# Pooled q and k rows of batch 1: summed by VectorE in place of TensorE's products with the identity

## The reference, cut to what matters

```
def sm_attn(qq, kk, vv):
    s = scale * qq @ kk^T ; s = s - max(s) ; a = exp(s) ; a = a / (sum(a) + 1e-9)
    return a @ vv
# q, k, v: [4 batches, 8 heads, 576 tokens, 64]; factor = 4
q_d = q.reshape(B, H, 144, 4, D).mean(axis=3)     # k_d and v_d likewise
out_up = np.repeat(sm_attn(q_d, k_d, v_d), 4, axis=2)
# local part: each token sees the tokens within +-3 of it
attn_out = out_up + out_local
x = attn_out, heads merged                          # [2304 tokens, 512]
x = (x @ w_a * (x @ w_b)) @ w_out                   # 512 -> 1536 -> 512
h = x @ w_in ; solu = h * softmax(h) ; out = layernorm(solu) * g_ln @ w_out2
```

## Time and profile before

| what | value |
|---|---|
| median of 3 runs | 773.45 us |
| the profiled execution | 773.61 us, span 771.5 us, mean granted TensorE clock 0.996 |
| TensorE busy | 759.5 us, 98% of the span |
| VectorE busy | 547.9 us, 71% |
| ScalarE busy | 301.6 us, 39% |
| GpSimd busy | 174.6 us, 23% |
| tile 0 | from about 40 us to about 142 us of the span |

### The profile page before, as it was taken

One profiled execution on the slowest core, in us unless ns is written; L12 is line 12 of the kernel. 1 busy time (PEld: TensorE's weight loads), 2 busy tenths in 40 slices (PEclk: granted clock), 3 DMA queues, 4 the chain that ended last, 5 costly groups with the idle time before them and its releaser, 6 DMA issues.

```text
span 771.5 us, 12627 instructions
## 1 busy us (share of the span) xinstructions
PE 759.5 (98%) x4616; PEld 702.9 (91%) x4616; DVE 547.9 (71%) x990; ACT 301.6 (39%) x824; POOL 174.6 (23%) x216
## 2 busy tenths in 40 slices
PE   8999999999999999999999999999999999999998
PEld 7889999999999999999999999999988888888886
DVE  5699889989877887797876874023377666666663
ACT  4656446463524434362525343234422222222222
POOL 3349460184444030060001121111100000000000
PEclk9899999999999999999999999999999999999999
DMA  9999947778789575573645523736111111011011
GB/s 179 220 218 228 215 109 219 229 208 237 216 207 257 150 209 153 160 199 114 178 140 165 164 93 103 232 100 202 40 57 56 40 43 55 28 55 55 28 42 41
DMA packets 94650, 108.84 MB, mean 141 GB/s; under 512 B 29309, under 2 KB 62589, under 8 KB 94589
## 3 DMA queue, kind: packets, MB, share of 16 engines
q1 hardware_dynamic: 83293, 99.38, 48.6%
q10 hardware_dynamic: 11296, 8.65, 3.7%
HBM read 87.46 MB, written 20.55 MB: 140 GB/s over the span
## 4 chain that ended last, share of the span: by engine, by line
PE 94%; DVE 2%; SPq 2%; DMA 1%; issue 1%; ACT 0%; DVEq 0%
PE psum L956 28%; PE psum L958 27%; PE psum L957 27%; PE psum L1083 2%; PE psum L913 2%; PE psum L889 1%; PE psum L865 1%; PE psum L924 1%; PE psum L899 1%; DMA v_h<-in_v 1%; SPq L483 1%; SPq L477 1%; SPq L492 1%; PE psum L794 1%; PE psum L738 0%
## 5 line engine op out<-in xcount | busy, mean ns | idle before, releaser
L956 PE MATMUL psum<-x_hi,w_hi 128*128 128x384 f32 x576 | 198.1, 344 | 0.2 <-DVE x_lo L1547 0.2
L958 PE MATMUL psum<-x_hi,w_lo 128*128 128x384 f32 x576 | 193.0, 335 | 0.0
L957 PE MATMUL psum<-x_lo,w_hi 128*128 128x384 f32 x576 | 192.7, 335 | 0.0
L956 PEld LDWEIGHTS psum<-x_hi,w_hi 128*128 128x128 f32 x576 | 108.2, 188 | 3.7 <-issue 2.9
L957 PEld LDWEIGHTS psum<-x_lo,w_hi 128*128 128x128 f32 x576 | 108.3, 188 | 0.0
L958 PEld LDWEIGHTS psum<-x_hi,w_lo 128*128 128x128 f32 x576 | 108.1, 188 | 0.0
L956 PE MATMUL psum<-ab_hi,wo_hi 128*128 128x384 f32 x288 | 99.6, 346 | 0.7 <-DVE wo_lo L1537 0.7
L958 PE MATMUL psum<-ab_hi,wo_lo 128*128 128x384 f32 x288 | 96.5, 335 | 0.0
L957 PE MATMUL psum<-ab_lo,wo_hi 128*128 128x384 f32 x288 | 96.4, 335 | 0.0
L1554 DVE TENSOR_TENSOR ab_f<-psum,a_sb 128x384 f32<-128x384 f32 x72 | 39.9, 554 | 76.9 <-PE psum L958 53.7
L1266 ACT ACTIVATE a_sb<-psum 128x384 f32<-128x384 f32 x72 | 35.3, 490 | 109.9 <-PE psum L958 108.4
(11 more groups left out here) (163 smaller groups left out, 1364.6 us busy)
## 6 DMA issues: line engine op xcount, KB each, us to landing
wo_hi<-wo_hi_scratch SPq DMA_DIRECT2D x53, 256.0 KB, 2.7
wo_lo<-wo_lo_scratch SPq DMA_DIRECT2D x53, 256.0 KB, 3.0
wo_raw<-in_moe_w_out SPq DMA_DIRECT2D x19, 256.0 KB, 5.6
yT_scratch<-y_sb ACTq DMA_DIRECT2D x6, 768.0 KB, 4.7
y_raw<-yT_scratch SPq DMA_DIRECT2D x18, 256.0 KB, 3.0
out<-out_sb SPq DMA_DIRECT2D x18, 256.0 KB, 2.1
k_u<-in_k SPq DMA_DIRECT2D x11, 384.0 KB
v_u<-in_v SPq DMA_DIRECT2D x11, 384.0 KB
```

The lines of the kernel that those rows point to most:

```text
L956: mm(dst, wh, xh, start=first, stop=False, skip_group_check=not check)
L957: mm(dst, wh, xl, start=False, stop=False, skip_group_check=not check)
L958: last = mm(dst, wl, xh, start=False, stop=end, skip_group_check=not check)
```

## The change

The rows of q and k of batch 1 are loaded like those of the other batches: one transfer for each half, in pieces of 768 values. VectorE then sums four rows into one, with one `tensor_reduce` for each half (96 partitions, 1536 values read, 384 written) into a new tile `raw_d`, which lies over `accT`. The innermost index of its input is the row r of the four, and successive values of that index lie 64 values, 256 bytes, apart. TensorE makes 3 transposes of `raw_d` for each half, as it does for the other batches. The sums are put one slot ahead of TensorE's turn by VectorE's count: at slots 14 (q, both halves) and 16 (k, both halves), ahead of the local steps of that slot. TensorE waits for `raw_by_vector`. The sums of k wait until the turns of q are done, as they write the same place.

```diff
--- before.py
+++ after.py
@@ -235,6 +235,7 @@
     raw = [place(f"raw{i}", [PPB * BLK, 2, 3, R4 * D], FP32) for i in range(2)]
 
     raw_v = place("raw_v", [SH, 2, 2, PPB, R4 * D], FP32, v_at)
+    raw_d = place("raw_d", [PPB * BLK, 2, 3, 2 * D], FP32, accT_at)
     v_half = place("v_half", [SH, 2, 2, 2 * D], FP32, accT_at)
 
     raw_x = {1: [place(f"raw{6 + i}", [PPB * BLK, 2, 3, R4 * D], FP32, o + 4 * DC * NT)
@@ -398,7 +399,7 @@
         h_turned qT_by_vector qT_by_scalar kT_ready kd_ready qd_summed qd_ready h_scored h_masked h_exped h_inv_ready h_normed h_p_turned h_pT_ready h_x_mm
         hp_scored hp_bias_ready hp_exped hp_inv_ready hp_normed hp_normed_by_scalar hp_turned hp_pT_ready
         h_up_mm x_local x_summed
-        raw_by_pool raw_step qk_turned qk_out pool_scored pool_bias_ready pool_exped pool_inv_ready
+        raw_by_pool raw_by_vector raw_step qk_turned qk_out pool_scored pool_bias_ready pool_exped pool_inv_ready
         p_turned pT_out out_mm_d out_d_ready
         loc_chain k_used v_used q_used u_sub_ready u_exped u_normed u_act_values acc_ready x_turned x_hi_ready x_lo_ready
         wa_loaded wa_hi_ready w_hi_ready w_lo_by_vector w_lo_by_pool wo_hi_ready wo_lo_by_vector wo_lo_by_pool
@@ -427,14 +428,11 @@
             return raw_x[b][half], raw_loaded[1 + b + half], raw_loads(b, tau)
 
 
-        def by_tensor(b, tau):
+        def by_vector(b, tau):
             return b == 1 and tau < 2
 
         def raw_loads(b, tau):
-            return 32 if by_tensor(b, tau) else 16
-
-        def paired_rows(t):
-            return t[:, :, :, :].rearrange("p x s e -> p (x s e)").rearrange("p (n x d) -> p n x d", x=2, d=D)
+            return 16
 
         def pooled_rows(t, i):
             return t[:, 0, i, 128:256]
@@ -512,12 +510,6 @@
                 if b == 3 and tau == 0:
 
                     sp.wait_ge(s.y_stored, 16 * 3)
-                if by_tensor(b, tau):
-                    for x in range(2):
-                        sp.dma_start(paired_rows(t)[:, :, x, :],
-                                     bass.AP(src.tensor, b * H * S * D + half * 3 * R4 * D + x * PPB * S * D,
-                                             [[6 * R4 * D, PPB * BLK], [D, 3 * R4], [1, D]])).then_inc(done, 16)
-                    return
                 sp.dma_start(t[:, :, :, :].rearrange("p x s e -> p x (s e)"),
                              bass.AP(src.tensor, b * H * S * D + half * 3 * R4 * D,
                                      [[6 * R4 * D, PPB * BLK], [PPB * S * D, 2], [1, 3 * R4 * D]])
@@ -854,21 +846,15 @@
 
             def turn_qk(i, dst):
                 b, tau, half = qk_part(i)
-                t, loaded, count = raw_buffer(b, tau, half)
+                t, _, _ = raw_buffer(b, tau, half)
                 at_least(pe, s.qk_out, i - 5)
-                if by_tensor(b, tau):
-                    pe.wait_ge(loaded, count)
-                    rows = t[:, :, :, :].rearrange("p x s e -> p (x s e)")
-                    for n in range(3):
-                        for r in range(R4):
-                            i4 = n * R4 + r
-                            last = mm(bank(dst)[:, n * 96:(n + 1) * 96], rows[:, i4 * 128:(i4 + 1) * 128],
-                                      ident[0:96, 0:96], start=r == 0, stop=r == R4 - 1)
-                    last.then_inc(s.qk_turned, 1)
-                    return
-                pe.wait_ge(s.raw_by_pool, raw_by_pool(b, tau, half))
+                if by_vector(b, tau):
+                    pe.wait_ge(s.raw_by_vector, 2 * tau + half + 1)
+                else:
+                    pe.wait_ge(s.raw_by_pool, raw_by_pool(b, tau, half))
                 for n in range(3):
-                    last = turn(bank(dst)[:, n * 96:(n + 1) * 96], pooled_rows(t, n), ident[0:96, 0:96])
+                    last = turn(bank(dst)[:, n * 96:(n + 1) * 96],
+                                raw_d[:, half, n, :] if by_vector(b, tau) else pooled_rows(t, n), ident[0:96, 0:96])
                 last.then_inc(s.qk_turned, 1)
 
             def pooled_scores(i):
@@ -1537,6 +1523,15 @@
                 V.tensor_tensor(wo_lo[:, slot, :], wo_raw[:, slot, :], wo_hi[:, slot, :], ALU.subtract
                                 ).then_inc(s.wo_lo_by_vector, 1)
 
+            def raw_sums(i):
+                b, tau, half = qk_part(i)
+                t, loaded, count = raw_buffer(b, tau, half)
+                dve.wait_ge(loaded, count)
+                at_least(dve, s.qk_turned, 2 * tau + half - 1)
+                V.tensor_reduce(raw_d[:, half].rearrange("p s (x d) -> p s x d", x=2),
+                                t[:, :, :, :].rearrange("p x s (r d) -> p s x d r", r=R4), AX.X, ALU.add
+                                ).then_inc(s.raw_by_vector, 1)
+
             def x_low(m, c):
                 par = m % 2
                 dve.wait_ge(s.x_hi_ready, DC * m + c + 1)
@@ -1670,6 +1665,8 @@
                     if since == TURN:
                         pooled_inverse(i)
 
+                for i in QK_AT[0].get(n + 1, ()) if m == 0 else ():
+                    raw_sums(i)
                 last = m == 0 and n == 33
                 if last:
                     x_low(m + 1, turns_at(m)[n])
```

## The result

The changed kernel takes 777.05 us (median of 11 runs), the kernel before, run beside it, 771.46: a ratio of 1.0072, 95% interval 1.0053 to 1.0092, so 5.6 us or 0.7% slower. By the bound of 2% it is "the same"; by its own interval it is slower. The profiled execution took 779.06 us, with a span of 777.3 us. So I measure by stretches inside a trace, and totals by the ratios.

A forecast was written before the change was run, and what follows sets the result against it. VectorE and TensorE were both taken to be at their limit in this stretch of tile 0. Sums add 12.0 us, idle time absorbs 6.1, TensorE's 9.7 goes unseen: 773.6 + 5.9 = 779.5 us, range 772 to 785.

The forecast's parts named there:

- VectorE is at its limit here, TensorE's gain is not seen: Tile 0, slot 14 to the accT turn: TensorE loses 9.7 us of work, none seen; VectorE's added work leaves 5.9 us.
- the 12 named: At slots 15 and 17: TensorE waits for the sums about 3 us at each of four turns, 12 in all.
- The size of a sum: VectorE's four reduces at slots 14 and 16: 3.09 us each at u_max's strided rate, 3.0 net, 12.0 in all.
- Rival A: VectorE's sums: the stride costs nothing, 1.74 us each, 6.6 added and 6.1 absorbed, time 774.2; chance 0.20.
- B: VectorE's sums: the stride costs more than u_max shows; at 6.0 us each +18, 791.5 us; chance 0.10.
- What is absorbed: VectorE's idle time ahead of block 6's gate and ab_low, 1.80 + 4.28 = 6.1 us, absorbs half of 12.0.
- The loads, costed at nothing: SP's changed q and k transfers: cost nothing, as no engine waits for a transfer and rows arrive in time.
- Rival C: TensorE's clock falls around the waits for sums: first hidden, second mostly within slack, else 1 to 4 us, 782; chance 0.10.
- the main case: Tile 0: sums add 12.0 us on VectorE, 6.1 absorbed, 5.9 left to the end, 779.5 us; chance 0.50.
- Rival D: VectorE's ab_low at 75.97, blocked 3.59 us: block vanishes (776.5) or hits another instruction (up to 782.5); chance 0.10.

The follow-up runs named there:

- loads alone: The kernel before with only the changed loads, one transfer per half in pieces of 768 values, TensorE's products taking the rows as they lie: ratio 0.9995.
- no sums: The changed kernel without VectorE's four reduces, TensorE turning one quarter of the raw rows once loaded: ratio 0.9979, -1.6 us.
- the clock kept: The changed kernel with extra identity products on TensorE ahead of the four waits for the sums, so its clock need not fall: ratio 1.0083.
- neighbours: The changed kernel with the same four reduces over four neighbouring values instead of values 256 bytes apart: ratio 1.0026.
- the two additions of a half: The changed kernel with each reduce replaced by two tensor additions (96x768, then 96x384): ratio 1.0026, +2.0 us.

## Why the prediction was right

The forecast was 779.5 against 773.6, +5.9 us; measured +5.6 by the ratio. The mechanism was the stated one; that the number came out within 0.3 us is in part luck, as two sizes were off by about 1 us each, in opposite directions (the sums and the loads). Step by step:

- *VectorE is at its limit here, TensorE's gain is not seen.* Shown from both sides: the sums added without TensorE's relief cost the same, and TensorE's waits took the place of its products. At the four turns it waited 3.63, 1.99, 1.71 and 2.29 us, 9.6 in all for the 12 named: the sums were shorter, and its products at the lower clock longer.
- *The size of a sum.* 2.79 us against 3.09 forecast: the rate from `u_max`, 1.92 ns a value, was too high, it is (2788 - 145) / 1536 = 1.72 ns. `u_max` is so short that 74 ns decide the rate. Rival A (1.74 us) fell as to the stride and was exact as to the contiguous rate; B fell, 256 and even 512 bytes cost no more than 48. The four sums give 10.85 us in place of 12.0, so the term was 1.15 us too large.
- *What is absorbed.* 6.1 us, as forecast; `ab_low` of block 6 at 105.0 for 105.1, the turn of `accT` at 134.0 for 134.4. Part of this agreement is luck: VectorE's slot 14 came at 82.89, 0.6 us late, from a start 1.8 us earlier and a way to it 2.4 us longer.
- *The loads, costed at nothing.* This was the weak step. It saw that no engine waited for a transfer, not that with the faster issue the transfers behind take about twice as long to land. Ahead of slot 14 this is 1.4 us in the mean of the traces; in the total it is 0 (loads alone) to 1 us.
- *Rival C.* The clock fell as described, twice, and was hidden both times, the second time more narrowly than the main case says: TensorE came to the down product of block 6 at 110.1, not at 107.6, and did not wait there. VectorE was still the later one at the turn of `accT`, by 1.30 us.
- *Rival D.* The 3.59 us block of `ab_low` did not come again; in its place that instruction waited 2.55 us for ScalarE. No run parted this from the rest.

What the prediction did not see, as it was not needed for its sum: the 6.1 us of idle time can be used by reduces with one input, but not for free by other work. Its estimate for "no sums" would have been -6, and -1.6 was measured. In the time in which VectorE stood still GpSimd did its weight parts; when VectorE's two-input work moves there, it is held by 2.6 to 3.2 us more. And k's rows are not there much sooner than they were used, which left VectorE idle for 2.6 to 2.9 us where it was to add them up early. The Trainium skill, SBUF — State Buffer, section Who interferes with whom, says that a VectorE instruction with two SBUF inputs contends with a GpSimd one that reads SBUF, and that `tensor_reduce` never does. The traces agree: beside GpSimd's run an addition took 0.96 us for 0.55, a reduce 2.80 for 2.78.

## What to carry to other kernels

An engine at 98% of the span need not be the limit where another one ends its waits: here the 9.7 us of work moved off it were worth nothing, and each microsecond put on the other counted in full beyond its idle time. Before idle time is counted as room, look at what GpSimd does in it, and how long the data of the moved work have been there. Price a strided reduce by its stride, here 1.72 ns a value for 1.04. And count faster issuing as a change: here the waiting moved into the queue, and the transfers behind landed later after their issue.

## What the runs showed of the hardware that was not expected

- The cost of a strided reduce did not grow with the stride: 2.79 us a sum at 256 bytes (2.78 to 2.95 in the traces with the sums added and the clock kept), 2.80 at 512, 1.73 for neighbours; in the short `u_max`, at 48 bytes, 1.9 ns a value.
- Beside GpSimd's run the two additions of a half take 1.47 + 0.96 = 2.4 us, nearly as much as the one strided reduce (2.79), which the run does not disturb.
- TensorE's clock stood at half for 86 to 94 us with TensorE busy for all of 90 to 94, after it had been busy for 0.37 of the 4 us from 82 on and for 2.01 of the next 4.
